# Head 0's copies ahead of the other loads in the prologue of clustered attention with two feed-forward layers

## The reference

```python
q_assign = argmax(einsum('bhsd,hcd->bhsc', q_n, c_n))    # cluster of each row, k_assign alike
mask = q_assign[:, :, :, None] == k_assign[:, :, None, :]
scores = where(mask, scale * q @ k.T, -1e9)
attn = exp(scores - max(scores)); attn = attn / (sum(attn) + 1e-9)
x = (attn @ v) as 1536 x 512
h = x @ w_in;  P = a0 + a1*h + a2*h^2 + a3*h^3;  Q = 1 + |b0|*|h| + |b1|*h^2
x = (P / (Q + 1e-6)) @ w_out
h = x @ w2_in;  out = (h - tanh(h)) @ w2_out
```

## Time and profile before

| | us |
|---|---|
| median of 3 runs | 792.02 |
| the runs | 788.97, 792.02, 792.41 |
| profiled execution, own time | 790.37 |
| its span | 788.6 |
| TensorE busy in it | 770.7 (98%) |

### The profile page before, as it was taken

The page is one execution under the profiler, slowest core; times in us unless marked ns, Lnnn a source line. Parts: engine busy times, 40 slices in busy tenths (PEclk is TensorE's granted clock), DMA queues, the critical chain, the costliest instruction groups (busy, mean ns, idle before and its releaser), DMA issues.

```text
span 788.6 us, 11292 instructions
## 1 busy us (share of the span) xinstructions
PE 770.7 (98%) x4006; PEld 664.4 (84%) x4006; DVE 502.7 (64%) x780; ACT 488.8 (62%) x936; POOL 286.1 (36%) x315
## 2 busy tenths in 40 slices
PE   6899999999999999999999999999999999999998
PEld 6799999899889878888888888888888888888886
DVE  5898989888888799999877888966211211111111
ACT  3788888888899788878766767776222322232222
POOL 3335545654667341222222212237322122222221
PEclk9999999999999999999999999999999999999999
DMA  8466566745631342000000020133000100010001
GB/s 193 98 163 164 138 157 162 175 119 140 164 101 51 107 155 81 0 1 1 1 0 1 25 83 27 55 116 124 1 0 1 54 0 1 1 54 0 1 1 53
DMA packets 66663, 54.66 MB, mean 69 GB/s; under 512 B 30736, under 2 KB 54832, under 8 KB 66608
## 3 DMA queue, kind: packets, MB, share of 16 engines
q1 hardware_dynamic: 66464, 53.91, 25.9%
q10 hardware_dynamic: 144, 0.03, 0.0%
HBM read 29.40 MB, written 3.19 MB: 41 GB/s over the span
## 4 chain that ended last, share of the span: by engine, by line
PE 83%; DVE 6%; POOL 3%; ACT 3%; issue 2%; DMA 1%; SPq 1%; POOLq 0%; ACTq 0%
PE y_ps L1256 33%; PE h_ps L1235 32%; PE pt_ps L1166 5%; PE s_ps L1155 5%; PE pv_ps L1189 5%; DVE pt_lo L934 3%; DVE nmax L921 2%; ACT pt_hi L649 1%; PE pr_ps L1087 1%; POOL xf L535 1%; PE pr_ps L1086 1%; ACT probs L642 1%; DVE qk_lo L848 1%; PE pr_ps L1117 1%; DMA qk_b<-qk_lo 1%
## 5 line engine op out<-in xcount | busy, mean ns | idle before, releaser
L590 POOL TENSOR_TENSOR g_lo<-f_t,g_hi 128x512 fp32r<-128x512 f32 x96 | 124.8, 1300 | 367.2 <-ACT g_hi L717 367.2
L1050 DVE TENSOR_TENSOR f_t<-h_ps,f_a 128x512 f32<-128x512 f32 x48 | 33.2, 691 | 203.4 <-ACT f_a L806 203.4
L1235 PE MATMUL h_ps<-x_lo,w_hi 128*128 128x512 f32 x384 | 149.6, 389 | 0.0
L1235 PE MATMUL h_ps<-x_hi,w_lo 128*128 128x512 f32 x384 | 149.5, 389 | 0.0
L1235 PE MATMUL h_ps<-x_hi,w_hi 128*128 128x512 f32 x384 | 149.5, 389 | 0.0
L717 ACT ACTIVATE g_hi<-f_t 128x512 fp32r<-128x512 f32 x96 | 60.8, 633 | 137.7 <-PE y_ps L1256 120.7
L934 DVE TENSOR_TENSOR pt_lo<-pt_ps,pt_hi 128x384 fp32r<-128x384 f32 x192 | 99.0, 551 | 30.1 <-ACT pt_hi L649 29.6
L649 ACT ACTIVATE pt_hi<-pt_ps 128x384 fp32r<-128x384 f32 x192 | 83.6, 489 | 27.8 <-PE pt_ps L1166 27.5
L921 DVE TENSOR_REDUCE nmax<-s_ps 128x1 f32<-128x768 f32 x96 | 91.0, 947 | 2.9 <-PE s_ps L1155 2.9
L642 ACT ACTIVATE probs<-s_ps,nmax 128x768 f32<-128x768 f32 x96 | 86.9, 905 | 2.4 <-DVE nmax L921 2.4
L1166 PE MATMUL pt_ps<-ident,probs 128*128 128x128 f32 x576 | 80.4, 276 | 4.6 <-DVE pt_lo L934 2.6
(11 more groups left out here) (141 smaller groups left out, 1476.4 us busy)
## 6 DMA issues: line engine op xcount, KB each, us to landing
w_raw<-in_moe_w_in_dram SPq DMA_DIRECT2D x32, 256.0 KB, 2.9
w_raw<-in_moe_w_out_dram SPq DMA_DIRECT2D x32, 256.0 KB, 3.2
ka<-qk_b SPq DMA_DIRECT2D x32, 192.0 KB, 3.9
raw_qk<-in_q_dram SPq DMA_DIRECT2D x16, 192.0 KB, 3.4
raw_qk<-in_k_dram SPq DMA_DIRECT2D x16, 192.0 KB, 4.1
raw_v<-in_v_dram SPq DMA_DIRECT2D x16, 192.0 KB, 2.6
qa<-qk_b SPq DMA_DIRECT2D x16, 192.0 KB, 4.0
qa<-qk_lo SPq DMA_DIRECT2D x16, 192.0 KB, 4.3
```

The lines of the kernel that those rows point to most:

```text
L590: pool.tensor_tensor(g_lo[n % 2][:, :], f_t[n % 2][:, :], g_hi[n % 2][:, :].bitcast(F32), ALU.subtract).then_inc(g_lo_done, 1)
L1050: dve.tensor_tensor(f_t[n % 2][:, :], h_ps[n % 4][:, :], f_a[n % 2][:, :], ALU.subtract).then_inc(g_done, 1)
L1235: last = pe.matmul(h_ps[n % 4][:, :], w[f][:, ws], x[:, cols], start=(kt == 0 and i == 0), stop=(kt == KT - 1 and i == 2))
```

## The change

The first loads are put in another order. SyncE copies head 0 (`spread(0)`) right behind the loads of heads 0 and 1, waits until all five copies have landed, and only then loads q and k of head 2, copies head 1, and loads v of head 0; v of head 1 follows at k = 2. Two of head 0's five copies, those from qk_lo, are issued on ScalarE's queue. The scaling of head 0's q goes from VectorE to ScalarE. On TensorE X0 of head 2 goes behind the first two score tiles, six identity products stand in its place, SIM of head 1 is cut in two halves around the score tiles, and head_0_hot takes its four groups in another order, the two of the keys in the middle. GpSimd ranks head 1 and finishes its one-hot rows before it splits v of head 0, and splits v of head 1 at k = 5, not 3. VectorE takes the row maximum of tile 0 before it reads head 1's similarities, and ScalarE the exponential of tile 0 before it copies head 2.

```diff
--- before.py
+++ after.py
@@ -218,8 +218,8 @@
                 "pt0": pt_ps[0][:, :], "pt1": pt_ps[1][:, :], "pv": pv_ps[:, :], "pr": pr_ps[:, :]}
         X0, X1, SIM, HOT, RZ = range(5)
         FIRST = 2
-        FIRST_UNITS = [(0, X0, "s0a"), (0, X1, "s0b"), (0, SIM, "pv"), (1, X0, "pt0"), (1, X1, "pt1"), (2, X0, "pr"),
-                       (1, SIM, "pv"), (2, X1, "pv"), (2, SIM, "pv")]
+        FIRST_UNITS = [(0, X0, "s0a"), (0, X1, "s0b"), (0, SIM, "pv"), (1, X0, "pt0"), (1, X1, "pt1"), (1, SIM, "pv"),
+                       (2, X0, "pr"), (2, X1, "pv"), (2, SIM, "pv")]
         first = [(g, u) for g, u, _ in FIRST_UNITS[:-1]]
         early_at = {k: [] for k in range(TILES)}
         late_at = {k: [] for k in range(TILES)}
@@ -235,7 +235,7 @@
         READ_AT = {1: 2} | {T * g - 12: g for g in range(3, HEADS)}
         TOP_AT = {k + 1: g for k, g in READ_AT.items()}
         TOP2_AT = {0: 1, 3: 2} | {T * g - 10: g for g in range(3, HEADS)}
-        FINISH_AT = {0: 1, 4: 2} | {T * g - 10: g for g in range(3, HEADS)}
+        FINISH_AT = {4: 2} | {T * g - 10: g for g in range(3, HEADS)}
         RZ_AT = [2 * T * p + 14 for p in range(PAIRS - 2)] + [TILES - 2 * T, TILES - 2]
         after_rz = {p: 3 if p < PAIRS - 2 else 0 for p in range(PAIRS - 1)}
         ROWS_OUT_AT = {2 * T * p + 13 + n: p for p, n in after_rz.items()}
@@ -365,6 +365,8 @@
                     sp.dma_start(ka[b][rows, :].bitcast(F32),
                                  qk_b[b][D:2 * D, 0, :].bitcast(F32)).then_inc(dup_in[b], 16)
                 sp.dma_start(qa[b][0:D, :].bitcast(F32), qk_b[b][0:D, 0, :].bitcast(F32)).then_inc(dup_in[b], 16)
+                if g == 0:
+                    return
                 sp.wait_ge(qk_lo_done, 2 * g + 2)
                 sp.dma_start(qa[b][D:2 * D, :].bitcast(F32), qk_lo[g % 2][0:D, :].bitcast(F32)).then_inc(dup_in[b], 16)
                 sp.dma_start(qk_b[b][0:D, 1, :].bitcast(F32),
@@ -402,11 +404,12 @@
             load_k(0)
             load_q(1)
             load_k(1)
+            spread(0)
+            sp.wait_ge(dup_in[0], spread_landed(0))
+            load_qk(2)
+            spread(1)
             load_v(0)
-            load_qk(2)
-            spread(0)
             load_qk(3)
-            spread(1)
             load_qk(4)
             spread(2)
             def swap_rows(hh):
@@ -441,7 +444,7 @@
                     g = (k + 2) // T + 1
                     sp.wait_ge(v_split, g)
                     load_v(g)
-                if k == 0:
+                if k == 2:
                     sp.wait_ge(v_split, 1)
                     load_v(1)
                 if k == 1:
@@ -562,8 +565,9 @@
                 pool.memset(rank[:, c:c + 1], float(C - c)).then_inc(rank_ready, 1)
             scale_q(1)
             scale_q(2)
+            rank_hot(1)
+            finish_hot(1)
             split_v(0)
-            rank_hot(1)
             scale_q(3)
 
             for k in range(TILES):
@@ -572,7 +576,7 @@
                     finish_hot(FINISH_AT[k])
                 if k in TOP_AT:
                     rank_hot(TOP_AT[k])
-                if r == 3 and 1 <= (k + 3) // T < HEADS:
+                if r == 3 and 2 <= (k + 3) // T < HEADS or k == 5:
                     split_v((k + 3) // T)
                 if r == 0 and 4 <= (k + 18) // T < HEADS:
                     scale_q((k + 18) // T)
@@ -691,6 +695,8 @@
                 act.activation(w_hi[c % NF][:, :], w_raw[c % NF][:, :], ACT.Copy).then_inc(w_hi_done, 1)
 
 
+            act.wait_ge(q_in[0], 16)
+            act.activation(raw_qk[0][:, :, 0, :], raw_qk[0][:, :, 0, :], ACT.Copy, scale=SCALE).then_inc(q_scaled_first, 1)
             copy_unit(0, X0)
             copy_unit(0, X1)
             act.wait_ge(cent_t, 1)
@@ -699,15 +705,18 @@
                 rows = slice(D * side, D * side + D)
                 act.activation(cq[rows, :, side, :, :], pr_ps[rows, 0:2 * P].rearrange("p (j h c) -> p h j c", j=2, h=H),
                                ACT.Copy).then_inc(cent_copied, 1)
+            act.wait_ge(qk_lo_done, 2)
+            act.dma_start(qa[0][D:2 * D, :].bitcast(F32), qk_lo[0][0:D, :].bitcast(F32)).then_inc(dup_in[0], 16)
+            act.dma_start(qk_b[0][0:D, 1, :].bitcast(F32), qk_lo[0][D:2 * D, :].bitcast(F32)).then_inc(dup_in[0], 16)
             copy_unit(1, X0)
             copy_unit(1, X1)
             act.wait_ge(dup_in[0], spread_landed(0))
             for half in range(2):
-                act.wait_ge(hot0_t, half + 1)
+                act.wait_ge(hot0_t, 3 * half + 1)
                 act.activation(qk_b[0][D:D + C, 0, half * HALF:(half + 1) * HALF], s_ps[1][D:D + C, half, 0:HALF],
                                ACT.Copy).then_inc(hot0_q, 1)
+            exp_tile(0)
             copy_unit(2, X0)
-            exp_tile(0)
             copy_unit(2, X1)
 
             def g_high(n):
@@ -849,9 +858,6 @@
                                   qk_b[g % QK_BUFS][:, 0, half_cols(u)].bitcast(F32),
                                   ALU.subtract).then_inc(qk_lo_done, 1)
 
-            dve.wait_ge(q_in[0], 16)
-            dve.tensor_scalar(raw_qk[0][:, :, 0, :], raw_qk[0][:, :, 0, :], SCALE, 1.0, ALU.mult,
-                              ALU.mult).then_inc(q_scaled_first, 1)
             dve.wait_ge(cent_act, 3)
             link(dve.tensor_scalar(c_st[:, 1:2], c_st[:, 1:2], 1e-30, None, ALU.add))
             link(dve.reciprocal(c_st[:, 2:3], c_st[:, 1:2]))
@@ -951,11 +957,11 @@
             qk_low(1, X0)
             qk_low(1, X1)
             head_0_keys()
+            row_max(0)
             read_sim(1)
             read_top(1)
-            row_max(0)
+            row_max(1)
             qk_low(2, X0)
-            row_max(1)
             qk_low(2, X1)
 
 
@@ -1091,7 +1097,7 @@
 
 
                 if u == SIM:
-                    if g < 3:
+                    if g in (0, 2):
                         similarities(g, 0)
                     similarities(g, 1).then_inc(prep_done, 1)
                     return
@@ -1121,10 +1127,8 @@
             def head_0_hot():
 
                 pe.wait_ge(hot0_zero, 2)
-                for i, bank in enumerate(("s1a", "s1b", "pt0", "pt1")):
-                    a, half = divmod(i, 2)
-                    if half == 0:
-                        pe.wait_ge(hot0_ready, a + 1)
+                for a, half, bank in ((0, 0, "s1a"), (1, 0, "pt0"), (1, 1, "pt1"), (0, 1, "s1b")):
+                    pe.wait_ge(hot0_ready, a + 1)
                     if a == 1:
                         wait_copied(pe, 1, (X0, X1)[half])
                     for t in range(HT):
@@ -1192,12 +1196,12 @@
                     last.then_inc(pv_done, 1)
 
             pe.wait_ge(ident_ready, 2)
-            def warm(count):
+            def warm(count, bank):
 
                 for i in range(count):
-                    pe.matmul(pt_ps[1][:, 0:P], ident[:, :], ident[:, :], start=True, stop=True)
-
-            warm(WARM)
+                    pe.matmul(BANK[bank][:, 0:P], ident[:, :], ident[:, :], start=True, stop=True)
+
+            warm(WARM, "pt1")
             unit(0, X0)
             unit(0, X1)
             pe.wait_ge(cent_ready, 1)
@@ -1205,16 +1209,18 @@
                 last = pe.transpose(pr_ps[:, part * P:(part + 1) * P],
                                     c_hl[:, part, :, :].rearrange("p a d -> p (a d)"), ident[:, :])
             last.then_inc(cent_t, 1)
-            warm(2)
+            warm(2, "pt1")
             pe.wait_ge(cent_copied, 2)
             unit(0, SIM)
             unit(1, X0)
             unit(1, X1)
-            unit(2, X0)
+            warm(6, "s0a")
             head_0_hot()
-            unit(1, SIM)
+            similarities(1, 0)
             score_tile(0)
             score_tile(1)
+            unit(1, SIM)
+            unit(2, X0)
             unit(2, X1)
 
             def hidden(n):
```

## The result

The changed kernel takes 794.15 us in the median of 10 runs (792.70 to 797.01), the kernel before 791.43 us in as many (788.97 to 792.51): a ratio of 1.0036, with a 95% interval of 1.0022 to 1.0050. That is 2.7 us more, where I had forecast 0.3 us less; it is outside my range. It lies inside the 0.5% that I called the limit of a measurement, but ten runs of each tell it apart: the limit was set too wide.

What follows compares the result with a forecast made beforehand. TensorE, busy 770.7 of 788.6 us, was taken as the bound, with score tile 6's wait deciding the change. 790.37 less 0.3 gave 790.1; the four times' average, 790.9, less 0.3 gave the forecast 790.6, range 788.3 to 792.9.

Steps and rivals of the forecast that it cites:

- the term of SyncE's queue: Seventeen issues ahead of head 1's one-hot copies, 0.73 us each, end at 24.9; tile 6 stays near 30.1.
- My rival of the second place: SyncE's queue behind head 2's late loads delays tile 6: 792.1 at 0.80 us an issue, 794.5 at 0.94; chance 0.22.
- the three signs that I had named for being wrong: Head 0's landing after 13.5, k of head 2 after 18, or one-hot copies over 1 us from 24.9 either way.
- My own estimate by bytes: SyncE's transfers ahead of head 1's one-hot copies: 3.3 MB from 13.9 on at 240 GB/s end at 27.7.
- Landing of head 0's copies: Last copy lands at 12.5 instead of 14.91, a gain of 2.4 us, of which 1.4 remains at score tile 0.
- Head 2: k lands at 17.3, up to 17.8; TensorE waits some 0.6 us; probability transposes start at 18.0, 0.9 us gained.
- The second queue: Two of head 0's copies on ScalarE's queue: worth at most two issues, 1.3 us; the bytes still set the landing.
- The products: Six identity products on TensorE, 9.95 to 11.4, counted as zero; what they guard is not shown to be needed.
- The clock rival: Pauses around 14.4 and 16.7 drop TensorE's clock to 1.2 GHz: about 792 to 796 us; chance 0.03.
- its comparison with the start: At the 1.2 GHz level TensorE's records would stand about twice as far apart, as they do at the start.
- GpSimd and v: v of head 0 split by about 24.3, of head 1 at about 33; all hidden, cover 4 us or more.
- From 40 us on: TensorE is full from 40 us on, and every shift is carried to the end.

Runs made afterwards that it cites:

- the kernel before with seven issues moved: The kernel before, with head 4's two loads and head 2's five copies issued behind head 1's one-hot copies: 794.16 us, 1.0034 of before.
- with seven issues moved: The changed kernel, with head 4's two loads and head 2's five copies issued behind head 1's one-hot copies: 794.92 us, 1.0054 of before.
- changed, again: The changed kernel unaltered, run again for a second profile and more timed runs: 794.06 us, 1.0052 of before.
- ten more products: The changed kernel with ten more identity products on TensorE in the stand ahead of score tile 6: 792.86 us, 1.0030 of before.
- no wait, head 4 late, again: Second run of the changed kernel without SyncE's landing wait, head 4's loads behind head 1's one-hot copies and v of head 1: 789.24 us, 0.9986 of before.

## Why the prediction was wrong

**The step that failed** is the term of SyncE's queue. I had its mechanism and its place: seventeen issues ahead of head 1's one-hot copies, a start later than 24.92 carried whole into tile 6. I sized an issue at 0.73 us, the mean of the kernel before, and put the result at 24.9. The issues took 14.3 us from 13.07 on, 0.84 each. The difference is in the four around 20.9 to 26.1: 2.08 us for k of head 4, 1.45 for a pair and 1.60 for one of head 2's copies, while the engines had a busy share of 1.19. My rival of the second place priced 0.80 an issue at 1.2 us; with 0.84 and a start 0.6 us later it gives 13.07 + 14.3 - 24.92 = 2.5 us, the measured 2.6 but for 0.1. Two of the three signs that I had named for being wrong came: k of head 2 after 18 us, and the one-hot copies more than 1 us late. My own estimate by bytes had warned of it: it ended at 27.7, where the full stretch now ends at 26.3, and I wrote "the same" and left the copies at 24.9. What I didn't weigh is that a queue behind full DMA engines is not a row of issues of fixed length: every issue that the wait delays is bunched with the rest. In the kernel before, the queue stood idle from 16.35 to 17.89 until TensorE had freed a buffer, and the engines caught up.

**Landing of head 0's copies.** Forecast 12.5, measured 13.05: the last of them took 4.97 us from its issue at 8.08, and ScalarE's queue was held by it for 1.20 us. Covered, as forecast. The 1.4 us at tile 0 came out as 1.2.

**Head 2.** Forecast 17.3 for k, measured 18.32; 0.5 us of it is the later landing, the rest the 4.62 us against 4.2. With it the transposes of probabilities came at 19.09 instead of 18.0, and the whole gain was gone well ahead of tile 6. I had 0.9 us left at this point.

**The second queue.** Counting it no further than the bytes was right; alone it brings nothing (1.0004). The rule of the Trainium skill, "DMA: Bandwidth & Descriptors", section "Issuing engines are not separate DMA queues", agrees with this run. Its remark that the sequencer's time to start a DMA is usually small relative to the DMA fits k of head 2, 0.65 of 4.62 us to the landing, and less so k of head 4 with the engines full, 2.08 of 7.6 us.

**The products.** Zero on the time is right. That they guard nothing is wrong: without them the stand is 2.07 us and not the 1.36 from which I argued, and the clock falls behind it. The clock rival had a chance of 0.03, for pauses of about 1 us "did nothing of the sort" in the one profile of before; yet the mean clock was under 0.999 in 58 of the 110 executions of the kernel before that the experiments timed. Nor does its comparison with the start fit: the first products took 0.24 us each, as did six transposes at 1.2 GHz (1.45 us, at 11.61 in the kernel before with seven issues moved), but the granted clock reads full at the start; I can't explain that.

**GpSimd and v.** Hidden in the changed kernel, as forecast (split of v of head 0 done at 25.2, of head 1 at 37.6). It has less cover than I gave it: with seven issues moved, the same late v of head 1 holds the queue for 5.0 us and stops tile 12.

**From 40 us on.** "Every shift is carried to the end" holds. Taking the start of tile 6 and TensorE's idle time from 60 to 300 us off the span leaves the same rest:

| profile | span | tile 6 | idle, 60 to 300 us | rest |
|---|---|---|---|---|
| before | 788.6 | 30.14 | 5.50 | 752.96 |
| changed | 793.8 | 32.75 | 8.29 | 752.76 |
| changed, again | 794.6 | 32.87 | 9.06 | 752.67 |
| ten more products | 790.1 | 32.22 | 5.23 | 752.65 |
| no wait, head 4 late, again | 787.4 | 29.57 | 5.78 | 752.05 |

In the four other profiles with a mean clock of 0.999 or 1.0 it is 752.4 to 752.9. By the medians the order is the same where nothing else moves: tile 6 at 29.5, 30.55, 30.72 and 32.8 goes with ratios of 0.998, 0.9995, 1.001 and 1.004. Where tile 12 stands too (29.6, with 1.005), and where the profiled execution is not typical (30.86, with 1.0036), it does not.

What stays open is the idle time from 60 to 300 us. It is 2.8 us more in the changed kernel than before, 3.6 us more in its second profile, and in both there is a wait of GpSimd near 80 us for the rows that go by way of DRAM (1.23 and 2.19 us). Both profiled executions are above their kernel's median, by 1.4 and 2.3 us, so most executions can't have it in this size, and with tile 6 as late as 32.22 it was 5.23, as before. A late tile 6 alone doesn't bring it about; whether it does now and then is not known.

## What to carry to other kernels

When transfers are held back to let one land early, follow the whole queue to the next latency-critical transfer, and price each issue by what it takes when the engines are full, not by its mean. The gain here came from taking two loads out of the way of six small copies that a tile waits for, not from the wait: in the changed kernel they were issued from 20.20 on, and head 4's q was first read at 37.59. Moving more behind them only shifts the stand to the next item that waits in the same in-order queue.

## What the runs showed of the hardware

An issue on SyncE's queue is not of fixed length: 0.59 to 0.65 us with room in the engines, up to 2.08 us in the changed kernel for one of 192 KB with them full. TensorE's granted clock fell to 1.2 GHz with single stands of 2.07, 2.65, 2.73, 2.78 and 3.42 us, but did not in two profiles behind 2.67 and 2.78 us. It also fell behind a stand of 1.11 us, and behind one of 0.96 followed by one of 0.59 us, where other profiles pass 1.05 and 1.36 us unharmed. So a stand of this length may or may not cost the clock. The low level lasted between 3 and 14 us, and the one fall that could be priced cost 1.55 us.
